# Another order for the start of a scan-and-MLP kernel: loads, squared rows and weight splits before its main loop

## The reference, cut to what matters

```python
k_n = k / (norm(k) + 1e-06)
for t in range(S):                                   # S = 768
    y[:, :, t] = einsum('bhd,bhde->bhe', q[:, :, t], state)
    v_old = einsum('bhde,bhd->bhe', state, kt)
    state = state + bt * einsum('bhd,bhe->bhde', kt, vt - v_old)
x = y as [3072, 384]
x = relu(x @ w_in) ** 2 @ w_out                      # 384 -> 2048 -> 384
x = max(x @ w1, x @ w2, x @ w3) @ w_out2             # 384 -> 768 -> 384
```

## Time and profile before

| | us |
|---|---|
| median of 3 runs | 946.07 (945.7 to 948.57) |
| the profiled execution, its device time | 946.07 |
| its span, first to last instruction | 944.1 |
| start of the first MLP matmul on PE | 104.30 |
| PE busy over the span | 868.9 (92%) |

### The profile page before, as it was taken

How to read it: one execution, slowest core, us unless ns; L and a number is a source line. 1 busy time by engine, 2 the same in 40 slices (tenths; PEclk the granted TensorE clock), 3 DMA queues, 4 the chain that set the end, 5 groups by cost and what they waited for, 6 DMA issues and landing times.

```text
span 944.1 us, 20905 instructions
## 1 busy us (share of the span) xinstructions
PE 868.9 (92%) x9148; PEld 743.6 (79%) x9148; DVE 428.9 (45%) x641; ACT 265.8 (28%) x464; POOL 285.4 (30%) x392
## 2 busy tenths in 40 slices
PE   2326699999999999999999999999999999999998
PEld 2326588878888888888888888887898989898988
DVE  6936365574566456645544444434323232323231
ACT  2211343233223322332233233633222222122221
POOL 4147898813941394139400000721000000000000
PEclk8658899999999999999999999999999999999999
DMA  7976764165424532353223134012020202010000
GB/s 185 220 142 148 160 148 102 52 138 132 106 60 97 131 105 60 93 129 80 64 63 91 36 95 123 9 51 67 1 67 1 67 1 67 0 67 1 34 1 34
DMA packets 123435, 76.27 MB, mean 81 GB/s; under 512 B 94320, under 2 KB 107120, under 8 KB 123344
## 3 DMA queue, kind: packets, MB, share of 16 engines
q1 hardware_dynamic: 121088, 73.89, 31.7%
q10 hardware_dynamic: 2256, 1.05, 0.4%
HBM read 53.18 MB, written 20.45 MB: 78 GB/s over the span
## 4 chain that ended last, share of the span: by engine, by line
PE 89%; DMA 3%; DVE 3%; SPq 3%; issue 1%; ACT 0%; ACTq 0%; DVEq 0%
PE psum L71 25%; PE psum L73 24%; PE psum L72 24%; PE psum L667 3%; PE psum L605 2%; PE psum L591 2%; PE psum L616 2%; PE psum L655 2%; PE psum L674 2%; PE psum L631 1%; PE psum L642 1%; DMA dram_f<-sol_f 1%; SPq L372 1%; DMA kz_first<-in_kT 1%; SPq L326 1%
## 5 line engine op out<-in xcount | busy, mean ns | idle before, releaser
L967 DVE TENSOR_TENSOR sq<-relu 128x512 f32<-128x512 f32 x96 | 76.2, 793 | 151.2 <-ACT relu L1103 151.1
L73 PE MATMUL psum<-x_lo,wb 128*128 128x512 f32 x324 | 126.3, 390 | 0.0
L72 PE MATMUL psum<-x_hi,wb 128*128 128x512 f32 x324 | 126.3, 390 | 0.0
L71 PE MATMUL psum<-x_hi,wb 128*128 128x512 f32 x324 | 126.2, 389 | 0.0
L71 PE MATMUL psum<-x_hi,win 128*128 128x512 f32 x288 | 116.3, 404 | 9.0 <-DVE x_lo L956 7.9
L1103 ACT ACTIVATE relu<-psum 128x512 f32<-128x512 f32 x96 | 57.3, 597 | 228.6 <-PE psum L73 228.6
L104 POOL TENSOR_TENSOR sol_tmp<-sol_b,sol_f 128x31 f32<-128x31 f32 (+15 forms) x155 | 90.1, 581 | 84.6 <-DMA sol_b<-dram_b 72.7
L71 PE MATMUL psum<-sq_hi,wout 128*128 128x512 f32 x288 | 114.2, 396 | 1.0 <-DVE sq_lo L972 1.0
L72 PE MATMUL psum<-x_hi,win 128*128 128x512 f32 x288 | 113.2, 393 | 0.0
L73 PE MATMUL psum<-x_lo,win 128*128 128x512 f32 x288 | 113.1, 393 | 0.0
L73 PE MATMUL psum<-sq_lo,wout 128*128 128x512 f32 x288 | 112.4, 390 | 0.0
(11 more groups left out here) (99 smaller groups left out, 1280.0 us busy)
## 6 DMA issues: line engine op xcount, KB each, us to landing
kz<-in_kT SPq DMA_DIRECT2D x40, 192.0 KB, 3.5
v_t<-in_vn SPq DMA_DIRECT2D x12, 384.0 KB, 3.5
qa<-in_qT SPq DMA_DIRECT2D x24, 192.0 KB, 3.8
nz<-in_kn SPq DMA_DIRECT2D x24, 192.0 KB, 4.3
x2T<-x SPq DMA_DIRECT2D x6, 768.0 KB, 4.1
x_raw<-x2T SPq DMA_DIRECT2D x6, 768.0 KB, 4.6
out_dram<-o_t SPq DMA_DIRECT2D x24, 192.0 KB, 1.9
raw_wb<-in_w SPq DMA_DIRECT2D x18, 192.0 KB, 4.4
```

The lines of the kernel that those rows point to most:

```text
L71: nc.tensor.matmul(out, lhs_hi, rhs_hi, start=first, stop=False)
L72: nc.tensor.matmul(out, lhs_lo, rhs_hi, start=False, stop=False)
L73: return nc.tensor.matmul(out, lhs_hi, rhs_lo, start=False, stop=last)
L967: nc.vector.tensor_tensor(d.sq[:], d.relu[:], d.relu[:], ALU.mult).then_inc(s.sq_ready, 1)
```

## The change

It touches the prologue alone, and three places of the first loop cycle on ACT.

- SP: rows for cycle 1, keys of chunks 2 and 3 and piece 0 are issued ahead of the first block stores; `store_beside(0)` and `(1)` ahead of `load_blocks(0)`; rows for cycle 2 and piece 1 directly behind it. The stores of chunks 2 and 3 (12 DMAs) and piece 3 come before `store_f(0)` instead of after it; piece 5 moves ahead of the second cycle's work.
- DVE: it clears `kz` instead of one `kz_first` tile; `sums(1)`, `norms(1)`, `take_kk(2)` and `take_kk(3)` stand ahead of the solve; `sums(1)` and `sums(2)` only add up, since POOL squares these rows.
- POOL: it clears all three `kz_first` tiles first and no longer waits for `cg_ready` 2; it squares two row tiles; `split_low(0)` and `(1)` no longer wait for `solved`.
- ACT: `root(1)` comes ahead of the splits, five pieces (`START_HI = 5`) are split before the loop instead of three, and the other three at f = 2, 4, 6 of the loop instead of f = 0 to 4.

```diff
-    START_HI = 3
+    START_HI = 5
@@ block.sync
             load_k_first(1)
-            load_v(0)
+            sp.dma_start(rows_of[1][:], kn[1]).then_inc(s.rows_in1, 16)
+            load_k_first(2)
+            load_k_first(3)
             sp.wait_ge(s.qa_zero, 1)
             load_q(0)
+            load_v(0)
+            load_piece(0)
             sp.wait_ge(s.cg_ready, 1)
             store_blocks(0, BLOCKS, s.b0_stored)
             sp.wait_ge(s.cg_ready, 2)
             store_blocks(1, BLOCKS[:2], s.b0_stored)
-            load_blocks(0)
-            load_swapped(0)
-            sp.dma_start(rows_of[1][:], kn[1]).then_inc(s.rows_in1, 16)
-            load_k_first(2)
-            load_k_first(3)
             store_beside(0, s.o0_stored)
             store_beside(1, s.o0_stored)
+            load_blocks(0)
+            sp.dma_start(rows_of[2][:], kn[2]).then_inc(s.rows_in2, 16)
+            load_piece(1)
             sp.wait_ge(s.nz_zero, 1)
             load_kn(0)
-            load_piece(0)
-            load_piece(1)
+            load_swapped(0)
             load_piece(2)
+            for c in (2, 3):
+                sp.wait_ge(s.cg_ready, c + 1)
+                store_blocks(c, BLOCKS, s.b_stored)
+                store_beside(c, s.o_stored)
+            sp.wait_ge(s.ob_zero, 3)
+            load_ob(0)
+            load_swapped(1)
             sp.wait_ge(s.qk_done, 1)
             load_k(1, True)
             load_v(1)
-            sp.dma_start(rows_of[2][:], kn[2]).then_inc(s.rows_in2, 16)
-            sp.wait_ge(s.ob_zero, 3)
-            load_ob(0)
+            sp.wait_ge(s.b_stored, B_TILE)
+            sp.wait_ge(s.o_stored, O_TILE)
+            load_piece(3)
             sp.wait_ge(s.kk_done, 4)
             load_piece(4)
             sp.wait_ge(s.fz_zero, 1)
             store_f(0)
             load_f1(0)
             load_fz(0, [1])
-            for c in (2, 3):
-                sp.wait_ge(s.cg_ready, c + 1)
-                store_blocks(c, BLOCKS, s.b_stored)
-                store_beside(c, s.o_stored)
             load_blocks(1)
             sp.wait_ge(s.x_done, 1)
             load_ob(1)
@@ block.gpsimd
-            nc.gpsimd.memset(d.kz[:], 0.0).then_inc(s.kz_zero, 1)
+            for t in first["kz_first"]:
+                nc.gpsimd.memset(t[:], 0.0).then_inc(s.kt_zero, 1)
...
-            pool.wait_ge(s.cg_ready, 2)
-            for t in first["kz_first"][1:]:
-                nc.gpsimd.memset(t[:], 0.0).then_inc(s.kt_zero, 1)
...
+            for n in (1, 2):
+                pool.wait_ge(rows_in[n], 16)
+                nc.gpsimd.tensor_tensor(rows_of[n][:], rows_of[n][:], rows_of[n][:], ALU.mult).then_inc(s.rows_sq, 1)
...
+            split_low(0)
+            split_low(1)
             pool.wait_ge(s.units_ready, 2)
             pool.wait_ge(s.solved, 1)
-            for i in range(3):
-                split_low(i)
+            split_low(2)
             solve(1)
@@ block.vector
             take_kk(1, 2)
+            sums(1, True)
+            norms(1)
+            take_kk(2, 4)
+            take_kk(3, 6)
             scale_v(0)
             dve.wait_ge(s.solb_in, 16)
             substitute(dve, nc.vector, s.dve_link, 2, ...)
-            sums(1)
-            norms(1)
-            take_kk(2, 4)
-            take_kk(3, 6)
             take_qk(0, 0)
+            scale_v(1)
             take_fd(0)
-            scale_v(1)
-            sums(2)
+            sums(2, True)
@@ block.scalar
+            root(1)
             for i in range(START_HI):
                 split_high(i)
             act.wait_ge(s.fs_stored, 16)
...
-            root(1)
             take_x(0, 4)
```

More of the change, by code:

```diff
@@ L222, in build @@
             "units_ready kz_zero kt_zero qa_zero fz_zero nz_zero sw_zero ob_zero mask_ready "
-            "beta_in rows_in0 rows_in1 rows_in2 rows_in ssq_ready root_ready norm_link c_ready cs_in "
+            "beta_in rows_in0 rows_in1 rows_in2 rows_in rows_sq ssq_ready root_ready norm_link c_ready cs_in "
             "kz_in kt1_in kt2_in kt3_in q_in kn_in v_in fz_in ob_in f1_in "
@@ L440, in _ @@
             load_kn(1)
[L441 to L444, removed]
+            sp.wait_ge(s.ssq_ready, 3)
+            load_piece(5)
+            load_swapped(2)
             sp.wait_ge(s.qk_done, 2)
@@ L450, in _ @@
             load_kn(2)
-            load_swapped(2)
-            for i in range(5, FIRST_WB):
-                load_piece(i)
+            load_piece(6)
+            load_piece(7)
             for i in range(CYCLES - 1):
@@ L821, in tile_cols, with sums @@
                 return slice(i * UNITS, (i + 1) * UNITS)
-            def sums(i):
-                if i < 3:
-                    dve.wait_ge(rows_in[i], 16)
-                else:
-                    dve.wait_ge(s.rows_in, 16 * (i - 2))
-                link(nc.vector.tensor_tensor(rows_of[i][:], rows_of[i][:], rows_of[i][:], ALU.mult))
+            def sums(i, squared):
+                if squared:
+                    dve.wait_ge(s.rows_sq, i)
+                else:
+                    if i == 0:
+                        dve.wait_ge(s.rows_in0, 16)
+                    else:
+                        dve.wait_ge(s.rows_in, 16 * (i - 2))
+                    link(nc.vector.tensor_tensor(rows_of[i][:], rows_of[i][:], rows_of[i][:], ALU.mult))
                 nc.vector.reduce_sum(d.ssq[:, tile_cols(i)], rows_of[i][:], AX_X).then_inc(s.ssq_ready, 1)
@@ L921, in attention @@
                     if h == at.sums:
-                        sums(i + 3)
+                        sums(i + 3, False)
                     if h == at.norms:
                         norms(i + 3)
-            nc.vector.memset(kz_of[1][:], 0.0).then_inc(s.kt_zero, 1)
+            nc.vector.memset(d.kz[:], 0.0).then_inc(s.kz_zero, 1)
             nc.vector.memset(zero, 0.0).then_inc(s.units_ready, 1)
@@ L930, in _ @@
             unit_matrix(dve, nc.vector, s.dve_link, 0, d.sol_f, zero, one)
-            sums(0)
+            sums(0, False)
             dve.wait_ge(s.beta_in, 16)
@@ L1117, in _ @@
                     attention(i, 2 * f + 1)
-                if i == 0 and f < FIRST_WB - START_HI:
-                    split_high(START_HI + f)
+                if i == 0 and f in (2, 4, 6):
+                    split_high(START_HI + f // 2 - 1)
                 if i == LAST and 3 <= f < 3 + KF2:
```

## The result

The changed kernel is slower. Its median over 15 runs is 953.52 us (950.68 to 958.72), that of the kernel before in the same job is 948.57 (944.88 to 952.72), and the ratio is 1.0062 with a 95% interval of 1.0047 to 1.0078: 0.6%, some 5 to 6 us (the two medians alone give 1.0052). The prediction said 947.1, in a range of 943.0 to 950.5, with "no change" as the likeliest. The time lies outside the range.

What follows compares the result with a forecast made beforehand. PE's matmuls bound the kernel from 104.30 us, so only the prologue's path can move: `y(0)` 1.6 us later, less 0.6 for the clock, gives +1.0 on 946.07, so 947.1 us, range 943.0 to 950.5.

Steps and rivals of the forecast that it cites:

- Start of the solve: Prologue, DVE: block stores queue behind three early load lots, so the solve starts at 28.7 instead of 21.19 us.
- 10.5 + 3 x 3.8 = 21.9: DMA queue: busy to about 10.5 us, then three lots at 3.8 each, so block stores get their turn at 21.9.
- rival 2: SP's queue, 10 to 28 us: block stores wait longer behind three lots, `sol_b` at 31.0, total 949.4 us; chance 0.24.
- Length of the solve: DVE in the prologue: POOL's multiplication and splits beside the solve hold its instructions, making it 10 us longer than 22.4.
- Rival 1: Solve in the prologue: POOL and DVE don't hold each other, total 943.5 us; chance 0.18.
- Solution to DRAM and back: After the solve: queue empty, so `dram_n` lands 3.1 us later, and the first `x_block` starts 3.2 us after that.
- `take_fd(0)` and `y(0)`: Prologue: `x_block(0)` to the end of `take_fd(0)` stays 12.05 us; `y(0)` follows without waiting, at 79.5 us.
- `y(0)` to the loop: End of the prologue on PE: same work as before, less 0.6 us for the clock; loop starts at 105.3 us.
- I count 0.6 back: `y(0)` on PE: without the 3.4 us idle time the clock no longer falls to half, gaining 0.6 us.
- The third rival: Clock around `f_d(0)`, `y(0)` and first MLP matmuls: 1.5 us won or lost, 945.6 to 948.6; within the forecast's 0.55.
- In the loop: Main loop: PE hardly waits and later pieces come no later, so nothing is added.
- Moved splits on ACT: nothing, hidden by the matmuls: First loop cycle on ACT: moved splits cost nothing under the matmuls, 1.7 us each without that cover.

Runs made afterwards that it cites:

- e1_splits_behind_solve: Changed kernel with POOL's splits of pieces 0 and 1 put back behind the wait for `solved`; median 951.32 us, ratio 1.0028 to the kernel before.
- c2_three_costs_out: Changed kernel with splits behind the solve, piece 0 loaded behind `sol_b` and loop splits at f = 2, 3, 4; median 949.31 us, ratio 0.9999.
- e5_loop_splits_early: Changed kernel with pieces 5, 6 and 7 split on ACT at f = 2, 3, 4 instead of 2, 4, 6; median 950.61 us, ratio 1.0010.
- e2_norms_free: Changed kernel with POOL waiting for cycle 0's norms on DVE before its later memsets and row multiplication; ratio 1.0065 to the kernel before.

## Why the prediction was wrong

**Direction and mechanism held, three terms did not.** The prediction's path was the one that counted: the solve late and long, the full queue's wait gone, the second `x_block` free. It gave +1.0 us, the two spans differ by 9.9, the medians by 5 and the ratio stands for 5.9.

- *Start of the solve: 28.7 predicted, 32.89 measured, +4.2.* The step that failed is "10.5 + 3 x 3.8 = 21.9", when the three lots are through and the stores' turn comes. The 10.5 was read from a busy share, 0.82 of 10 us. The tile view of before has the real number: the two loads of `qa` issued at 5.1 and 5.6 land up to 6.4 us later, so at 12.0, and three lots start there.

```profile
L304 SPq DMA_DIRECT2D qa<-in_qT x2: 422/425/428, 5.1 to 5.6; - x2
...
DMA to landing us min/median/max: 5.8/6.1/6.4
```

In after ACT splits piece 0 at 25.08, as it lands, (25.1 - 12.0) / 3 = 4.4 us per lot. From there to the issue of `sol_b` it is 3.6 us, against 3.5 for eight stores, but that agreement is luck. Two of the eight go out on ACT's queue (from 17.80), the last one is issued at 24.9 and lands at 28.2, and what SP does last before it gets to `sol_b` is to issue the four off-diagonal stores (`dram_o`, 26.55 to 28.66), which the prediction had left out. `sol_b` itself took 4.2 instead of 3.3; why is open, but it took 4.0 in e1_splits_behind_solve too, and 3.3 in both profiles of before. So +1.5 from the queue's end, +1.7 from the lots, +0.1 from the stores, +0.9 from `sol_b`. The queue moved 192 GB/s at full share in that stretch, not the 231 of the earlier trace rows, on which the lower bound of 3.4 rested. That was rival 2, at a chance of 0.24; its mechanism is the right one and its 31.0 was still 1.9 short. By the other four profiles with this order a lot took 3.7 to 4.4 us and the solve started at 30.65 to 33.18, so part of the +4.2 is this execution's; the queue's end and `sol_b` are off in all of them.

- *Length of the solve: 10 predicted, 9.0 measured.* Right, in size and in manner (just one instruction passes between two of POOL's). The multiplication took 2.75, the low end of the bounds, against 3.4 taken. Rival 1 is refuted. The multiplication and the splits are 10.3 us of POOL in place of the 10.9 that were added up. The rule of the Trainium skill that the prediction named there (page SBUF — State Buffer, section "Who interferes with whom") holds in these rows.

- *Solution to DRAM and back: right.* 3.1 predicted, 2.7 measured, and 2.8 to the first `x_block` against 3.2. "The queue is empty as the solve ends" held, in part by luck, since the solve ended 3.2 us later than predicted: in e1_splits_behind_solve, with its end at 55.6, the queue was busy to about 60, and in c2_three_costs_out, to 62. The 60.6 that I had for it was near.

- *`take_fd(0)` and `y(0)`: right.* 12.15 against 12.05 and no wait in front of `y(0)`. It started at 82.11 against 79.5: 4.2 from the start of the solve, less 1.0, 0.4 and 0.4 in the steps named above, and 0.2 more in this one.

- *`y(0)` to the loop: 25.8 predicted, 29.2 measured.* "I count 0.6 back" was true of `y(0)`, which took 2.09, and was taken away again by `y(1)`, which took 3.68 at a granted clock of 0.50. Before's second profile has the same row. Of the 3.4 us 1.5 are the clock behind `y(1)` (10.0 to 11.5 from there to the loop), which differs between before's own two profiles as well; 0.6 are the gain that was counted; and 1.3 are the way from `y(0)` to `y(1)`, 17.7 instead of 16.4, which the prediction took as "the same work in the same order". Most of these go away with piece 5 late. The third rival, the clock, had the right size, 1.5 either way.

- *In the loop: 0 predicted, 2.9 measured between the two spans, and 3.5 won back in e5_loop_splits_early.* "Moved splits on ACT: nothing, hidden by the matmuls" is the other step that failed, and no rival covered it. ACT's 1.7 us is hidden, true. But a split on ACT is half of a hand-over: POOL takes the other half, in order, and has its solve behind it. The delay had to be followed from ACT to POOL (13 us of waiting, a solve that ends 7 us later against the loop) and from there to the norms of the cycle boundary (2.07 us instead of 0.17) and to PE's idle 3.7 us.

The base was off as well. "946.07, which is also the median" was the median of three; of fifteen it is 948.57. With the terms as measured the sum of +1.0 gets 2.6 more up to `y(0)`, 1.5 more to the loop (+0.9 against before's second profile instead of -0.6) and 2.9 behind it: 8.0, where the ratio's interval stands for 4.5 to 7.4. The rest is scatter of single executions that I can't assign.

## What to carry to other kernels

When a chain of short instructions is the path, price every multiply or split that POOL does beside DVE's chain at its full duration (9.0 us lost for 10.3 here), and look at each moved load as so many us in front of every later transfer, from the landing of the last one before it and not from the busy share. Follow a moved half of a hand-over to the engine that takes the other half, and to what that engine has queued behind it. And once a wait is cut, read off the next bound before counting the gain: here the queue came free some 3 us before the solve ended, so taking 11 us from one gave 2.5.

## What the runs showed of the hardware that I had not expected

- A DVE instruction with a single SBUF input waited for POOL too, and for instructions of POOL that only write. `TENSOR_SCALAR` on 128x32 took 1.04 and 0.98 us in after beside POOL's `MEMSET`s, and 0.18 in e2_norms_free without them; 2.07 beside a POOL multiply, 0.17 in e5_loop_splits_early. Two `TENSOR_TENSOR` with two inputs each, at 10.63 and 10.86 beside the same `MEMSET`s of after, took 0.19. The Trainium skill, page SBUF — State Buffer, section "Who interferes with whom", has both halves: an instruction with one input stays clear of GpSimd only outside the modes that use both ports, and `tensor_scalar` may enter such a mode. The rows agree with that; the prediction had looked only at the two-input rule.
- SP's issues themselves take longer behind a full queue: four `dram_b` issues took 5.25 us in after and 8.20 in e2_norms_free, where they begin 3.4 us earlier behind the same lots, against 2.42 in before, where the queue was slack.
- One full lot more or less in front moved the start of the solve by 3.6 us on average, but an earlier issue behind the same lots changed next to nothing: 3.4 us earlier gave 0.8, and profiles with the same order differ by 2.5.
- The same kernel, at the same place to the hundredth of a us, ran `y(1)` in 2.09 us in one execution (granted clock 1.00) and in 3.68 in another (0.50).
